# Attention, gated MLP and squared-ReLU MLP in one kernel: constant matrix products placed ahead of TensorE's waits in the coarse attention stage

## What is computed

```
q_d, k_d, v_d = means over groups of 4 positions        # 144 x 64 for each head
out_up    = repeat(softmax(scale * q_d @ k_d.T) @ v_d, 4)
out_local = softmax(where(|i - j| < 4, scale * q @ k.T, -1e9)) @ v
x = out_up + out_local                                  # 2304 x 512
xn = x / sqrt(mean(x * x) + 1e-6) * rms_g
y = (silu(xn @ w_gate) * (xn @ w_val)) @ w_out          # d_ff 1536
h = relu(y @ w_in);  out = (s * h * h + b) @ w_out2     # d_ff 2048
```

## Time and profile before

| | us |
|---|---|
| median of 3 runs | 986.19 |
| lowest and highest | 985.36, 987.17 |
| the profiled execution | 982.59 |
| its span, first to last instruction | 980.8 |
| TensorE busy | 950.3 (97%) |
| VectorE busy | 539.6 (55%) |
| ScalarE busy | 355.4 (36%) |
| GpSimd busy | 369.8 (38%) |
| mean granted TensorE clock | 0.944 of full |

### The profile page before, as it was taken

How to read it: one execution, slowest core, us unless ns; L and a number is a source line. 1 busy time by engine, 2 the same in 40 slices (tenths; PEclk the granted TensorE clock), 3 DMA queues, 4 the chain that set the end, 5 groups by cost and what they waited for, 6 DMA issues and landing times.

```text
span 980.8 us, 12959 instructions
## 1 busy us (share of the span) xinstructions
PE 950.3 (97%) x4863; PEld 774.8 (79%) x4891; DVE 539.6 (55%) x815; ACT 355.4 (36%) x816; POOL 369.8 (38%) x192
## 2 busy tenths in 40 slices
PE   4799999999999999999999999999999999999998
PEld 3799899767777777777778998888888888888897
DVE  6899997876774765554532323434433443343343
ACT  2458845753225222422241434222222322222232
POOL 5757867777882876356600454000000000000000
PEclk8555599999999999999999999999999999999999
DMA  9897672533321231012003332102001100100010
GB/s 249 221 262 243 185 224 83 160 94 110 101 84 38 83 108 46 20 33 75 14 27 113 126 124 65 43 1 87 1 1 43 43 0 1 65 1 1 1 43 23
DMA packets 54379, 79.41 MB, mean 81 GB/s; under 512 B 9836, under 2 KB 37068, under 8 KB 52908
## 3 DMA queue, kind: packets, MB, share of 16 engines
q1 hardware_dynamic: 52284, 71.53, 24.8%
q10 hardware_dynamic: 2032, 7.05, 1.9%
HBM read 67.05 MB, written 11.50 MB: 80 GB/s over the span
## 4 chain that ended last, share of the span: by engine, by line
PE 82%; DVE 6%; DMA 4%; ACT 3%; issue 2%; POOL 1%; SPq 1%; ACTq 0%; DVEq 0%; POOLq 0%
PE bank L779 23%; PE bank L919 7%; PE bank L920 7%; PE bank L921 7%; PE bank L903 7%; PE bank L902 7%; PE bank L901 7%; PE bank L815 4%; PE bank L813 4%; PE bank L814 4%; PE bank L1898 2%; PE bank L1865 2%; DMA rawq<-in_q_dram 1%; DVE sc L594 1%; PE bank L1850 1%
## 5 line engine op out<-in xcount | busy, mean ns | idle before, releaser
L549 POOL TENSOR_TENSOR prod<-qs,ks 128x896 f32<-128x896 f32 x80 | 178.1, 2250 | 83.2 <-DVE sc L594 60.3
L563 POOL TENSOR_TENSOR prod<-sc,vs 128x896 f32<-128x896 f32 x72 | 136.5, 2003 | 66.5 <-DVE x L604 34.7
L942 DVE SCALAR_TENSOR_TENSOR r<-bank,r 128x512 f32<-128x512 f32 (+1 forms) x80 | 51.1, 638 | 180.9 <-ACT r L930 180.9
L903 PE MATMUL bank<-y_h,w2i_l 128*128 128x512 f32 (+1 forms) x320 | 117.7, 368 | 0.0
L930 ACT ACTIVATE r<-bank 128x512 f32<-128x512 f32 (+1 forms) x80 | 44.4, 555 | 181.8 <-PE bank L903 181.1
L835 DVE TENSOR_TENSOR bank<-bank,u 128x512 f32<-128x512 f32 (+1 forms) x66 | 39.6, 600 | 120.9 <-PE bank L779 115.8
L813 PE MATMUL bank<-h_h,wo_h 128*128 128x512 f32 (+1 forms) x264 | 102.7, 389 | 0.0
L779 PE MATMUL bank<-x_h,wv_h 128*128 128x512 f32 (+1 forms) x264 | 100.4, 392 | 0.0
L594 DVE TENSOR_REDUCE sc<-prod 128x14 f32<-128x896 f32 x80 | 85.7, 1078 | 15.7 <-POOL prod L549 15.6
L815 PE MATMUL bank<-h_h,wo_l 128*128 128x512 f32 (+1 forms) x264 | 93.3, 353 | 0.0
L814 PE MATMUL bank<-h_l,wo_h 128*128 128x512 f32 (+1 forms) x264 | 92.5, 350 | 0.0
(11 more groups left out here) (136 smaller groups left out, 1941.3 us busy)
## 6 DMA issues: line engine op xcount, KB each, us to landing
raww<-in_moe_w_out_dram SPq DMA_DIRECT2D x14, 512.0 KB, 4.1
ks<-in_k_dram SPq DMA_DIRECT2D x16, 280.0 KB
vs<-in_v_dram SPq DMA_DIRECT2D x16, 280.0 KB, 5.6
y_scr<-y_st ACTq DMA_DIRECT2D x4, 1024.0 KB, 5.3
raww<-in_moe_w_in_dram SPq DMA_DIRECT2D x8, 512.0 KB, 3.6
y_raw<-y_scr SPq DMA_DIRECT2D x4, 1024.0 KB, 4.9
out_dram<-o_st SPq DMA_DIRECT2D x16, 256.0 KB, 2.8
rawq<-in_q_dram SPq DMA_DIRECT2D x3, 1152.0 KB, 14.2
```

What stands on the lines that cost most here:

```text
L549: pool.tensor_tensor(dst, qv, kv, ALU.mult).then_inc(prod_ready, 1)
L563: pool.tensor_tensor(dst, pv, vv, ALU.mult).then_inc(prod_ready, 1)
L903: last = pe.matmul(o, w2i_l[:, m, kk, :], y_h[t % 2][:, kk, 0:w], start=False, stop=kk == DT - 1)
```

## The change

TensorE gets additional products that nobody reads. Their operands are constants in SBUF, 128x128 weights over 512 columns in bf16, and they overwrite a PSUM bank that the work behind them overwrites again.

- 12 of them at the start, on `junk`, which DVE fills with ones as its first instruction (semaphore `fill_made`). They stand ahead of TensorE's first wait.
- 3, 3 and 2 behind the second, fourth and sixth unit of batch 0's transposes, on the identity read as bf16.
- In the loop, `keep_running(bank, count)` ahead of the wait on the turned k (for n of 1 and more) and ahead of the wait on the exponents of head n-2. The count is 3 up to n = 8 and 1 from n = 9 on.

In all that is 12 + 8 + 47 + 46 = 113 additional products, and one memset. The waits on `ctr_evac` and `cpt_evac` ahead of the transposes of exponents now stand before the wait on `cexp`; the set of waits is the same.

```diff
+RUNNING = (3, 1)
...
+            dve.memset(junk[:, :], 1.0).then_inc(fill_made, 1)
             dve.memset(kT[D:JH, :, :], 0.0)
             dve.memset(qT[D:JH, :, :], 0.0).then_inc(pad_made, 1)
...
+            pe.wait_ge(fill_made, 1)
+            for _ in range(12):
+                pe.matmul(CSC[0][:, :], junk[:, 0:P], junk[:, :], start=True, stop=True)
             pe.wait_ge(consts_made, 4)
+            ones = ident[:, :].bitcast(BF16)
+            def keep_running(o, count):
+                for _ in range(count):
+                    pe.matmul(o[:, :], ones[:, 0:P], over(ones, [[0, 2], [1, 2 * P]]), start=True, stop=True)
...
             for i in range(UNITS):
                 turn_pooled(0, i)
+                if i % 2:
+                    keep_running(CSC[0], 3 if i < UNITS - 1 else 2)
             for n in range(HEADS + VAL_LAG):
                 if n < HEADS:
...
                     wait(pe, cexp, 2 * (n - 2))
+                    if n:
+                        keep_running(CSC[n % 3], RUNNING[n > H])
                     pe.wait_ge(ctr_evac, UNITS * b + (UNIT if b else UNIT0).index(("k", third)) + 1)
...
                 if TURN_LAG <= n < HEADS + TURN_LAG:
                     g = n - TURN_LAG
+                    wait(pe, cpt_evac, g - 1)
+                    pe.wait_ge(ctr_evac, UNITS)
+                    keep_running(CPT[g % 2], RUNNING[n > H])
                     pe.wait_ge(cexp, 2 * (g + 1))
-                    pe.wait_ge(ctr_evac, UNITS)
-                    wait(pe, cpt_evac, g - 1)
```

## The result

The change made the kernel slower: 987.59 us in the median of 18 runs (984.29 to 993.75) against 985.38 for the kernel before (18 runs, 982.42 to 987.17) on the same chip. The ratio is 1.003, with a 95% interval of 1.0017 to 1.0042. 983.3 was forecast. The time is inside the stated range (980 to 993), on the side that had been given 0.29.

The account below looks back on a forecast made before the run. VectorE's list was taken to set the coarse stage's pace, waiting 4.0 us for TensorE's scores at half clock. Gains of 1.12 + 1.5 + 0.28 = 2.9 us turned 986.19 into 983.3 us, range 980 to 993.

Parts of the forecast that it names:

- the side that had been given 0.29: Whole kernel: chance 0.29 of being slower than before by more than 2 us, the difference a measurement can tell.
- the clock holds: TensorE in the coarse stage: constant products, the densest work it has, keep the full clock; the prediction said this decides.
- the sum of 2.9 us: Coarse stage: 1.12 us at head 8, 1.5 at three short stalls and 0.28 at the end, off VectorE's list.
- Case A: Coarse stage: the clock stays up and VectorE's waits shrink; 983.3 us, own range 980 to 985.2, chance 0.50.
- Rival B: Coarse loop: clock falls in gaps, products cost more than they bring; 992 us, from 988 to 1004, chance 0.30.
- the prediction's argument against B: Late heads: each head at half clock adds dense work, so TensorE gets busier and the clock comes back.
- The stall of head 8: VectorE's 2.46 us wait at 39 us: 1.12 us gained at full clock; bounds a 0.4 loss to 2.46.
- The three short stalls, 1.5 us: VectorE's waits for scores at heads 15, 23 and 27: all 1.5 us go, TensorE being ahead at full clock.
- rival C: VectorE's lead is lost to loads, through GpSimd's wait for k: 0 to 1.5 us gain, 985.5 us, chance 0.15.
- the last sentence of the prediction: VectorE's list: forecast wrong if its own instructions take longer beside others of GpSimd than before; no size given.
- Start and end: Start products cost 0; at the end VectorE gains 0.28 us, TensorE's further 3.0 us lost at transposes of x.

Follow-up runs that it names:

- second profile of before: The unchanged kernel run once more to get another profile of it; 986.63 us in one run.
- Small products: The changed kernel with its loop and between-unit products as fp32, 72x72 weights, 256 columns; 1018.73 against 984.74 us for before, ratio 1.0326.
- Three late, wait filled: The changed kernel with 3 products in all heads and 8 more ahead of the wait for batch 1's k means; 984.64 against 984.88 us for before.
- half the work: The kernel before with about half of TensorE's coarse-stage work left out and no products added; 986.18 against 984.88 us, ratio 0.9995.
- after again: The changed kernel run once more, unaltered, for a second profile; 986.02 us in one run.
- third profile: The changed kernel run a third time, unaltered, for its profile; 986.88 us in one run.
- Loop only: The changed kernel with only the loop's products, without the junk fill and the products at the start; 990.97 against 984.01 us for before, ratio 1.007.
- late products only: The kernel before plus one product ahead of each of the two waits from head 9 on, nothing else; 986.9 against 983.61 us, ratio 1.0025.
- six and three: The changed kernel with 6 products ahead of each wait up to head 8 and 3 from head 9; 989.03 against 984.74 us for before, ratio 1.0039.
- fill only: The kernel before plus only the memset of junk and TensorE's wait on it, no products; 985.4 against 984.01 us, ratio 1.0008.

## Why the prediction was wrong

Two steps failed: that the clock holds, and, even where it does, the sum of 2.9 us.

**Does the clock hold?** Case A had 0.50 on a clock that stays up. In the three profiles of after it fell five, four and three times from the coarse stage on, for 37.5 to 51 us in all, counted to the rise behind each fall. Its mean was 0.968 to 0.978 in all 18 runs. Every fall in the coarse stage of the kernels with products came in a standstill of TensorE of 0.88 us or more or at most about 2 us behind one; not every such standstill brought one. The prediction had seen that the products run ahead of a wait and not during it; it took the dense work between as enough against that. It also misread the fall at 17.1 us as one among short standstills. The fall lies in a standstill of 2.16 us that began at 16.80, as the empty window at 17.1 in the earlier trace rows hints:

```profile
18.96 1.19 PE L1898 MATMUL bank<-dv,cpT 72*72 72x64 f32 x8 [2.16 <-DVE dv L1543]
```

And the rise at 13.7 us behind transposes, on which it let them help, didn't repeat in the second profile of before. The Trainium skill's page "TensorE: Matmul & The Clock Gate" (section HAM oscillation) has bursts between waits go back to the lower clock each time. The trace agrees in kind, and not in each case: one wait of 2.2 us brought a fall at 36.8 us in one execution and none in two others.

**Rival B** had the mechanism: stretches at half clock, 3.24 us a head in them, VectorE waiting for scores at their end. Its least price was 988 on a scale where before stood at 986.19, 1.8 us more; measured were 2.2. Its likeliest, 992, was too high, since it counted ten heads in one stretch beyond what VectorE can cover. The long stretches took four to six heads each and ended by themselves, as the prediction's argument against B had said: each slow head brings dense products. "Small products" show the other case.

**The stall of head 8.** The term was 1.12 us, on condition of full clock. With it the stage from 3 to 8 gave 15.11 - 13.90 = 1.2. Without it the bound was a loss of 0.4; measured was 0.2. Both ends of the term are right; which one comes differs between executions of the same program, and in the first profile it was the loss.

**The three short stalls, 1.5 us.** This term of the sum is wrong also with the clock up. "Three late, wait filled" and "half the work" have a quick TensorE, and what they gain behind head 8 is what is left of the whole gain once the stage from 3 to 8 is taken out: 0.4 - (15.11 - 14.49) = -0.2 us in the one, 1.9 - (15.11 - 13.98) = 0.8 us in the other. In their place VectorE waits for GpSimd's products, ScalarE's `prod_a` and loads of v, between 0.2 and 1.6 us each. That is rival C's mechanism: the waits that went were closely followed by others.

**VectorE's own instructions.** The sum moves VectorE's list by its waits alone and takes its instructions as fixed; the last sentence of the prediction named the danger. `vd` ran three times in each of the 16 profiles. It took 0.76 us in the 24 cases in which no product of GpSimd was under way as it began, and 2.13 to 2.53 us in the 24 in which one was. A wait that goes moves VectorE's instructions against GpSimd's, so some of them get longer or shorter by more than the stalls in question. In "after again" and the third profile that is 0.9 us lost, in "half the work" 2.5 us gained. How much of it is chance of the order isn't shown.

**Start and end.** The start cost nothing that can be told, as forecast, though for a reason that was half of it: the products ahead of the scores of heads 1 and 2 were not counted, cost VectorE 0.4 or 1.3 us (by which profile of before one takes) and seem to have been taken up by the wait for the load of q. That TensorE's lead behind the coarse stage is given back at the transposes of x could not be tested. It waited there, after

```profile
PE bank L727 <- DVE x_l L760: 2.0, 2, 1.7
PE bank L727 <- ACT x L708: 1.6, 1, 1.6
```

3.6 us, against 2.5 in the first profile of before, but the second profile of before has more than either:

```profile
PE bank L724 <- DVE x_l L757: 4.8, 3, 1.9
```

**What stays open.** The 2.02 us that after's first profile waited for the load of k of batch 2 (line 1004):

```profile
58.96 1.36 DVE L1004 TENSOR_TENSOR rawk<-rawk 128x1152 f32<-128x1152 f32 x1 [2.02 <-DMA rawk<-in_k_dram]
```

"Loop only", "late products only" and "six and three" waited 1.24, 0.39 and 0.74 us there; the other two profiles of after, and both with three late products, not at all, nor did any kernel that has no late products. Why that load is sometimes late isn't shown. Nor is it shown what decides, for the same wait, whether the clock falls, or why a product of GpSimd that is under way makes `vd` three times as long.

## What to carry to other kernels

Before work is added to raise TensorE's clock, ask who would finish earlier: here another engine set the pace, all but 4 us of TensorE's time was covered, and the shorter waits among those 4 us were closely followed by others. Compare the busy time of the engine that sets the pace as well as its waits: the same instructions can take longer once they fall beside another engine's. Profile the same kernel more than once before a stage is explained. A filler ahead of a wait doesn't fill the wait; it must be long enough to end as the wait ends, and placed at the waits where the engine really stands still. Its price must be carried at the lower clock too, where it is double: here it was paid there in part of the heads.

## What the runs showed of the hardware

TensorE that is busy without any gap doesn't get its full clock by that: with small products it was busy 95.00 of 95 us at 0.50. In "late products only" the clock came up from half at 43.4 us, soon after the first heads with two products of 128x128 weights over 512 columns (0.86 of 3.25 us of a head's work), where before stayed at half. A clock that had fallen in the coarse stage of after came back 3.4 to 24 us later in its three profiles.

The addition `vd` of VectorE (128x576 of fp32) took 0.76 us, and 2.13 to 2.53 us when a product of GpSimd was under way as it began, in 24 cases of each. GpSimd's products beside it took 2.4 to 3.3 us, where the means of the two kinds are 2.25 and 2.00 us in before.

In after the clock fell once more in the MLP, behind the transposes of x, and the gate products took 0.43 us each there instead of 0.23. The window of that stretch:

```profile
217.80:221.00 3.20, 3.20 (x9) 1.93 (x9) 2.54 (x4) 0.90 (x2) 2.39 (x2) 0.50 0.00 0
```

Such a fall, of 3.4 us, came between 216 and 228 us in five of the profiles, two of them of kernels without products in the loop ("fill only" and "half the work"), and at 252.2 us in "small products". Its cost wasn't isolated.

A product of fp32 with 72x72 weights over 256 columns is two instructions in the trace ("small products", 93.93 us) and takes 0.86 us at half clock, as much as two bf16 products of 512 columns (0.43 us each).
